# An attention and mixture kernel: the attention step in another order on TensorE and VectorE, the splits spread over steps, the router product in column groups, filler products before the expert tiles

## The reference

```python
def phi(x):
    proj = np.einsum('bhsd,df->bhsf', x, w_phi)
    proj = proj - np.max(np.abs(proj), axis=-1, keepdims=True)
    return np.concatenate([np.exp(proj), np.exp(-proj)], axis=-1)
q_p, k_p = (phi(q), phi(k))                     # q, k, v: (4, 8, 576, 64)
kv = np.einsum('bhsf,bhsd->bhfd', k_p, v)
z = np.sum(k_p, axis=2)
num = np.einsum('bhsf,bhfd->bhsd', q_p, kv)
den = np.einsum('bhsf,bhf->bhs', q_p, z)[..., None] + 1e-06
x = num / den                                   # as (4, 576, 512)
...
gate = 1.0 / (1.0 + np.exp(-gate_pre))          # causal convolution of x, 5 taps
y = gate * (x @ w_val) @ w_out
...
logits = np.einsum('bsd,de->bse', y, w_gate)    # e: argmax, or that of the token before
out[b, s] = p[e] * (np.maximum(y[b, s] @ w1[e], 0.0) @ w2[e])
```

## Time and profile before

| | us |
|---|---|
| three executions | 593.65, 594.37, 596.05 |
| median | 594.37 |
| profiled execution, its own time | 596.32 |
| its span, first to last instruction | 594.6 |
| start to step 1 | 0 to 31.7 |
| steps 1 to 15 | 31.7 to 188.8 |
| products with w_val, four batches | 188.8 to 240.5 |
| logits, y, scatter | 241 to 299 |
| rows back, expert tiles | 306 to the end |

### The profile page before, as it was taken

How to read it: one execution, slowest core, us unless ns; L and a number is a source line. 1 busy time by engine, 2 the same in 40 slices (tenths; PEclk the granted TensorE clock), 3 DMA queues, 4 the chain that set the end, 5 groups by cost and what they waited for, 6 DMA issues and landing times.

```text
span 594.6 us, 12965 instructions
## 1 busy us (share of the span) xinstructions
PE 554.7 (93%) x5189; PEld 469.4 (79%) x5189; DVE 310.2 (52%) x491; ACT 268.5 (45%) x463; POOL 216.9 (36%) x218
## 2 busy tenths in 40 slices
PE   4999999999979999999949999999999999999994
PEld 4888878787868999678838888888888888888883
DVE  3276776767686555285424555621456665542121
ACT  2245556564566621363524556522456555532221
POOL 2019898989979930437410100010000011000100
PEclk9999999999989999999979999999999999999998
DMA  8233635535440000008924665531356666411110
GB/s 308 89 119 119 197 98 180 165 106 187 129 153 2 1 1 2 0 1 247 290 101 139 216 239 167 195 106 53 96 187 192 207 210 208 141 39 49 35 52 21
DMA packets 30231, 75.04 MB, mean 126 GB/s; under 512 B 3311, under 2 KB 3439, under 8 KB 30192
## 3 DMA queue, kind: packets, MB, share of 16 engines
q1 hardware_dynamic: 23536, 58.73, 30.9%
q0 software_dynamic: 3200, 9.46, 4.2%
q10 hardware_dynamic: 3456, 6.32, 3.9%
HBM read 57.94 MB, written 17.61 MB: 127 GB/s over the span
## 4 chain that ended last, share of the span: by engine, by line
PE 90%; DVE 2%; ACT 2%; issue 2%; DMA 2%; POOL 0%; ACTq 0%; SPq 0%; POOLq 0%; DVEq 0%
PE turn L507 10%; PE turn L508 10%; PE turn L509 10%; PE num_ps L507 7%; PE num_ps L508 7%; PE num_ps L509 7%; PE pair_ps L516 6%; PE kv_ps L550 6%; PE num_ps L563 6%; PE pair_ps L697 3%; PE pair_ps L507 3%; PE pair_ps L509 3%; PE pair_ps L508 3%; PE turn L492 2%; PE turn L502 2%
## 5 line engine op out<-in xcount | busy, mean ns | idle before, releaser
L469 POOL DMA_INDIRECT out_rows<-o_sb,meta_cur x22 | 25.5, 1159 | 262.9 <-DVE o_sb L1112 262.9
L443 POOL TENSOR_TENSOR gate<-gate,tap 128x576 f32<-128x576 f32 x64 | 93.1, 1454 | 5.3
L1103 DVE TENSOR_TENSOR h_t<-pair_ps,h_t 128x512 fp32r<-128x512 f32 x44 | 30.4, 692 | 115.3 <-ACT h_t L899 115.3
L967 DVE TENSOR_TENSOR wts<-stage,wts 128x1024 fp32r<-128x1024 f32 x64 | 75.7, 1218 | 10.9 <-ACT wts L842 10.9
L507 PE MATMUL num_ps<-wts,y_t 128*128 128x512 f32 x176 | 72.6, 412 | 1.5 <-DVE y_t L1094 1.5
L507 PE MATMUL turn<-wts,h_t 128*128 128x512 f32 x176 | 73.2, 416 | 0.0
L842 ACT CAST wts<-stage 128x1024 fp32r<-128x1024 f32 x64 | 65.1, 1048 | 12.7 <-PE turn L509 11.1
L508 PE MATMUL num_ps<-wts,y_t 128*128 128x512 f32 x176 | 70.5, 401 | 0.0
L509 PE MATMUL num_ps<-wts,y_t 128*128 128x512 f32 x176 | 70.4, 400 | 0.0
L508 PE MATMUL turn<-wts,h_t 128*128 128x512 f32 x176 | 69.7, 396 | 0.0
L509 PE MATMUL turn<-wts,h_t 128*128 128x512 f32 x176 | 69.6, 395 | 0.0
(11 more groups left out here) (158 smaller groups left out, 1045.7 us busy)
## 6 DMA issues: line engine op xcount, KB each, us to landing
stage<-in_w SPq DMA_DIRECT2D x64, 512.0 KB, 4.6
kq_t<-in_kq SPq DMA_DIRECT2D x16, 576.0 KB, 6.0
sorted_rows<-padrow SPq DMA_DIRECT2D x9, 771.0 KB, 5.8
ysl<-sorted_rows ACTq DMA_DIRECT2D x24, 257.0 KB, 2.7
v_sb<-in_v_aug SPq DMA_DIRECT2D x16, 325.0 KB, 3.1
wout_t<-in_w_out_t SPq DMA_DIRECT2D x1, 1024.0 KB, 8.1
wval_sb<-in_w_val SPq DMA_DIRECT2D x1, 1024.0 KB, 10.1
wout_sb<-in_w_out SPq DMA_DIRECT2D x1, 1024.0 KB, 12.3
```

The source lines that it names most:

```text
L443: nc.gpsimd.tensor_tensor(g, g, tap[:, t % 2, :], ALU.add).then_inc(conv_step, 1)
L967: nc.vector.tensor_tensor(lo, whole, hi.bitcast(F32), ALU.subtract).then_inc(signal, 1)
```

## The change

The step on PE gets another order (`TURNS` is 4, with a group that holds both mixed slabs, of q of pair n and of the output of n-1, and is turned last); the mixed products are those of pair n+2; the numerators take the mixed slab last. In front of the loop the mixed products of pairs 0 and 1 are made. DVE's step is `shift` for k of n+1, `normalise` of n-1, `shift` for q of n+1, `shift` for the mixed slab of n+2. The loop has two rounds (steps 1 to 8), and steps 9 to 15 are written out. Each of them from 9 on ends with one rounding on ACT, and DVE makes its rest at the start of the next one; the last two rests of `w_val` stand behind the last `normalise`. `wog` is made as four groups of 32 rows of one bank, and turned inside step 0. `w_out` is loaded in step 1. Before and behind `turn_y(0)` there are 26 and 5 products of constants whose result nobody reads.

The core of the diff (left out: places in SBUF, the writing-out of counters, ACT's functions, which follow PE's order):

```diff
-    TURNS = 5
+    TURNS = 4
...
-        LOOPS = (PAIRS - 4) // 4
-        PADS = 3
+        LOOPS = 2
+        PADS = 9
...
+        def splits():
+
+            return {9: [("x", 0)], 10: [("x", 1)], 11: [("x", 2)], 12: [("x", 3)], 13: [("w", 0)],
+                    14: [("w", 1)], 15: [("w", 2), ("w", 3)]}
...
+                if n == 3:
+                    sp.wait_ge(wog_made, 1)
+                    sp.dma_start(wout_sb[:], w_out.rearrange("(c p) n -> p c n", p=P)).then_inc(wout_in, 16)
...
+                if left >= 1:
                     project_k(n + 1)
-                for j in range(3):
+                for j in range(2):
                     turn_q(n, j)
...
                 if not first:
-                    for j in range(2):
-                        turn_x(n + (-1), j, number_of(n, 3 + j))
-                pe.wait_ge(kvz_ok, n.times(1, 1))
-                numerators(n)
-
+                    turn_x(n + (-1), number_of(n, 2), turn_ps[0])
+                turn_mixed(n, first)
+                if left >= 2:
+                    project_mixed(n + 2)
+                if first:
+                    turn_wog()
+                numerators(n, first)
...
+                for kk in range(CT):
+                    for c in range(CT):
+                        ins = nc.tensor.matmul(num_ps[c * LGW:(c + 1) * LGW, 0, 0:P], wg[:, kk, :],
+                                               wout_t[:, kk, c * P:(c + 1) * P], start=(kk == 0), stop=(kk == CT - 1))
+                ins.then_inc(wog_made, 1)
...
+            def keep_going(count):
+
+                for _ in range(count):
+                    nc.tensor.matmul(kv_ps[:, 0:P], ones[:], lower[:], start=True, stop=True)
+
+            keep_going(26)
             turn_y(0)
+            keep_going(5)
...
+            def step(n, left):
+
+                if left >= 1:
                     shift(1, n + 1)
+                if not (isinstance(n.loop, int) and n.k == 0):
+                    normalise(n + (-1))
+                if left >= 1:
                     shift(2, n + 1)
-                normalise(n)
+                if left >= 2:
+                    shift(0, n + 2)
...
             for n in last_pairs():
-                step(n, last=(n.k == PAIRS - 1))
...
+                for what, c in split_in.get(n.k - 1, []):
+                    rest_of_x(0, c) if what == "x" else rest_of_wval(c)
+                step(n, PAIRS - 1 - n.k)
+            normalise(Step(0, PAIRS - 1))
+            for what, c in split_in.get(PAIRS - 1, []):
+                rest_of_wval(c)
```

More of the change, by code:

```diff
@@ L565, in numerators @@
                 ins.then_inc(num_ok, 1)
-            def step(n, first=False, last=False):
-                if not last:
+            def step(n, left):
+                first = isinstance(n.loop, int) and n.k == 0
+                if left >= 1:
                     project_k(n + 1)
-                for j in range(3):
+                for j in range(2):
                     turn_q(n, j)
@@ L622, in _ @@
                     if b == 0 and i == 1:
-                        for j in range(2):
-                            turn_x(Step(0, PAIRS - 1), j, TURNS * PAIRS - 2 + j, last=True)
+                        turn_x(Step(0, PAIRS - 1), ALL_TURNS - 2, turn_ps[0])
+                        bank_free(ALL_TURNS - 1)
+                        turn_x_mixed(turn_ps[1]).then_inc(turned, 1)
             pe.wait_ge(gated_ok, B * 2 * CT)
@@ L797, in _ @@
-            step(Step(0, 0), first=True)
+            step(Step(0, 0))
             with act.Fori(0, LOOPS) as g:
@@ L948, in normalise, with step @@
                 ins.then_inc(normed, 1)
-            def step(n, first=False, last=False):
-                if not last:
-                    shift(0, n + 1)
+            def step(n, left):
+                if left >= 1:
                     shift(1, n + 1)
+                if not (isinstance(n.loop, int) and n.k == 0):
+                    normalise(n + (-1))
+                if left >= 1:
                     shift(2, n + 1)
-                normalise(n)
+                if left >= 2:
+                    shift(0, n + 2)
             shift(0, Step(0, 0))
```

260 lines of the change are left out of this document (145 added, 115 removed).

## The result

The changed kernel takes **576.14 us** (median of four executions, 575.43 to 577.15) against 594.37, a ratio of 0.969 with a 95% interval from 0.967 to 0.971. The profiled execution took 575.43, with a span of 573.7. The forecast was 578.3, with a range of 573.0 to 585.0.

A forecast was written before the change was run, and what follows sets the result against it. TensorE, busy for 93% of the span, was taken to bound the kernel; 8.4 + 0.2 + 4.8 + 2.7 = 16.1 us off the profiled 596.32 gave 580.2, and 1.95 less for the median gave 578.3 us, range 573.0 to 585.0.

The forecast's parts named there:

- gap: PE idle before the first w_val product, waiting for the last two splits behind the last normalise: 4.1 us.
- hole: PE's wait of 6.96 us before the first row tile, with half rate after it; fillers to gain 2.7 us.
- Part 1: Loop steps 1 to 9: mixed slab turned last, step 10.28 to 9.35 us, gain 8.4 us.
- The cover of normalise: Loop step: normalise ends 0.2 us before PE's turns of the previous output need it, a thin cover.
- Part 2: Steps 10 to 15: splits one per step; gains 0.5 and 6.3, losses 4.1 and 2.5, sum 0.2 us.
- Part 3: Start: router product 6.99 to 2.1 us, step 1 at 26.9 against 31.70, gain 4.8 us.
- Part 4: Before the first row tile: filler products keep PE's clock at full rate, gain 2.7 us (0 to 3).
- A: Clock does not fall before the w_val products, or split steps last 9.65: some 574 us; chance 0.12.
- B: PE waits some 0.55 us for normalise or a bank every step, loop step 9.9: 583 us; chance 0.15.
- C: Fillers before the first row tile do not keep the clock, or end late: 581 us; chance 0.08.
- D: k/q loads come too late for the mixed products made ahead: 617 us, slower than before; chance 0.03.
- E: Loop step keeps its length as banks are freed late; only start and row-tile wait gain: 587 us; chance 0.02.

The follow-up runs named there:

- the longer normalise: The changed kernel with the two products over num_ps in normalise made twice, the first into a spare tile: 584.75 us.
- the one line moved: The kernel before with only the turns of the mixed slab's features moved behind the sums, ahead of the query projection: 579.70 us, ratio to before 0.976.
- the start filled: The 566.76 us version (rests behind DVE's step, all before the last normalise) plus four and six filler products at the start: 566.78 us.

## Why the prediction was right, point by point

The sum had 16.1 us and the profiled executions differ by 20.9; 18.2 by the medians, since the profiled execution was the slowest one before and the fastest one after. The median of 576.14 is 2.2 below the forecast and well inside the range. By its own parts, from the profiled executions:

| part | forecast | measured | from |
|---|---|---|---|
| 1: loop, steps 1 to 9 | +8.4 | +9.0 | 92.41 before, 83.39 now |
| 2: steps 10 to 13 | +0.5 | +0.9 | 41.18, 40.32 |
| 2: step 14 | +6.3 | +6.3 | 15.94, 9.64 |
| 2: step 15 and gap, idle time and all | -4.1 | -3.8 | 7.56, 11.38 |
| 2: half rate behind the gap | -2.5 | -1.5 | twelve products, 0.24 apart |
| 3: start, to step 1 | +4.8 | +7.0 | 31.70, 24.72 |
| 4: hole | +2.7 | 3.1 | without the fillers |

**Part 1** was right in mechanism and size. The step is 9.16, not 9.35: the mixed products next to the numerators save 0.16 (0.59 and 2.25 from start to start before, 0.49 and 2.19 now), where I took 0.05, and the held turn gives 0.81 from start to start, not 0.74. The cover of normalise was put at 0.2; it ends at 104.31 (103.74 + 0.57) and the turn starts at 104.62, so it is 0.31, and the longer normalise confirmed it. One stall of 0.73 in step 3, which no part had, hides some of the gain. What the experiments add is which part of the new order does it: the turn of the mixed slab behind the sums, alone, brings 10.28 to 9.46; the rest of it 0.3 more, in turns and mixed products that stand next to others of their kind.

**Part 2** held in its sizes. A step with a split is longer than a loop step by as much as was said, but the wait stands in two places and not one: in steps 11 to 13, 0.50 at the turns of the output and 0.32 at the q projection, which waits for the late subtraction of k and which the sum did not have. The gap is 3.63 and not 4.1, because its two rests took 1.14 and 0.68 and not 1.10 each. DVE and POOL there:

```profile
167.65 1.14 DVE L1035 TENSOR_TENSOR wval_lo<-wval_sb,wval_hi 128x512 fp32r<-128x512 f32 x1
...
168.72 0.68 DVE L1035 TENSOR_TENSOR wval_lo<-wval_sb,wval_hi 128x512 fp32r<-128x512 f32 x1
```

```profile
166.84 1.41 POOL L455 TENSOR_TENSOR gate<-gate,tap 128x576 f32<-128x576 f32 x1
168.22 1.71 POOL L451 TENSOR_SCALAR tap<-x_t,conv_sb 128x576 f32<-128x576 f32 x1
```

The Trainium skill, "GPSIMD Engine Reference", key points, has POOL contend for SBUF with DVE instructions that have two SBUF inputs. The trace agrees, and shows who pays: the first rest starts while an instruction of POOL runs and ends 0.54 behind it (168.79 and 168.25); the second takes 0.68 with POOL just as busy, and POOL's instruction beside it takes 1.71 where the same one took 0.75 at 166.01. So 0.68 is not the price with POOL idle alone, as the prediction had it, and the median of four stands for no single rest: two rests took 1.74 here, 2.63 and 2.50 in other kernels. That the gap came out near was partly luck. The clock did fall. Its cost was over-sized: 1.5 us. What the prediction did not see is how poor the changed splits are. It compared them with before; with only the one line moved, step 14 takes 11.52 (151.86 to 163.38), so 4.4 of the 6.3 can be had with the old splits where they meet POOL as they did there.

**Part 3** is the step that was mis-sized, by 2.2 us. The product was put at 2.1 and starts 1.87 ahead of the next one. Step 0 was put 16.9 to 26.9 and ran from 15.07 to 24.72. Of the difference, 0.7 is the first load, which landed earlier in this execution (5.34 against 6.04), and 0.9 the q projection ahead of the product, which took 1.16 and not 2.08; the rest is 0.2 in the product and 0.35 in step 0. The first two differ between executions of kernels with the same start, so 1.6 of the 2.2 is luck of this execution and not a gain of the change. The old product put back cost 7.3 by the medians and 6.5 in the trace, near the 7.0 of this part. Behind it the clock stayed at 0.50 through the k projection, the turns and the sums (2.08, 1.97, 3.22), longer than in the trace of before (2.08, 1.34, 2.53), which the prediction had measured from.

**Part 4**: 26 products last 5.97 (6.2 was said) and end before the rows land; the wait that is left is 1.23, and that for DVE 0.38 in place of 1.49. Leaving the fillers out cost 3.1.

**The rivals.** A (the clock does not fall in the gap, or split steps of 9.65; 574) fell: it is at 0.50 in 170 to 172, and those steps take 10.13. B fell for this kernel, and the longer normalise shows how near it was. C fell with the experiment on the fillers. D: the waits have no k/q load but the first. E: the loop step is shorter by all that was said.

## What to carry to other kernels

Where one engine waits at the same place in every step, move that one instruction behind the next independent block before rewriting the order: here one line gave 14.6 of 18.2 us, some 10.7 of it in steps 1 to 13, and it changed what the rest of the rewrite was worth. Where two engines slow each other, read the cost of an instruction from rows at the place where it will stand: the same two took 1.74 to 2.63 us. Put work that waits for a slow helper behind what the busiest engine needs from its engine, never in front, and end such a row of side work one step before its consumer. An idle stretch of the matrix engine can have two prices, its length and the slow products behind it; a filler saves the second only where no other engine sets the pace.

## What the runs showed of the hardware that I had not expected

- A wait of 1.94 us at the end of the old splits left the granted clock at 1.00, as did one of 1.86 in step 3 of the start filled; one of 2.67 at the place of the first was followed by 0.50, as were gaps of 3.63 and 4.52, and the stall of 2.10 in step 3 without fillers.
- PE can stall for 0.5 to 2.1 us with no releaser in the trace while a packet of instructions is late behind large DMA writes; the stall moved from 47 to 160 us with them.
- A subtraction of two SBUF tiles of 128x512 on DVE took 0.68 to 1.90 us with POOL busy beside it, and POOL's one-input instruction 0.75 or 1.71.
- 16 fp32 products (32 instructions) with weights of 32 columns in four column groups take 1.94 us at a granted clock of 0.50 and 1.08 at 1.00; the same result with weights of 128 columns and 9 moving columns takes 7.00 at 0.50.
- The start is where executions differ: in the profiled ones the q projection at 11 us took 1.16 in some and 2.08 in others of kernels with the same start, and with the old router product the executions spread over 7.7 us.
